# Attention by halves of a batch, woven into the chunks, and the token mix from chunk 7 on

## The chip, the cores and the metric

The kernel runs on one core of a Trainium2 chip. The metric is the device time of one execution in microseconds (us), the median of several runs; lower is better. TensorE (PE) does the matrix products, VectorE (DVE) and ScalarE (ACT) work on what it leaves in PSUM, GpSimd (POOL) has no PSUM work here, and SyncE (SP) issues every DMA.

## The reference, cut to what matters

Four batches of 576 tokens; 8 heads of 64 columns.

```python
scores = q @ k.T / sqrt(64)                      # per batch and head, 576 x 576
rel = pos[:, None] - pos[None, :]
plain   = (rel >= 0) & (rel < 32)                # heads 0 to 3
dilated = (rel >= 0) & (rel < 128) & (rel % 4 == 0)   # heads 4 to 7
attn = softmax(where(mask, scores, -1e9)); x = attn @ v          # B, S, 512

xk = mu_k * x + (1 - mu_k) * x_prev; xr = mu_r * x + (1 - mu_r) * x_prev   # first block
x2 = sigmoid(xr @ w_r) * (relu(xk @ w_k) ** 2 @ w_v)             # 512 -> 1024 -> 512

u = x2 + (x2.T @ U @ V).T                        # second block: token mix, rank 32
out = u + relu(u @ w_ch1) @ w_ch2                # 512 -> 2048 -> 512
```

Only 32 keys count for a query. A dilated head is a plain one once the tokens are sorted by their residue mod 4 (144 tokens each).

## The kernel before, in words

**Precision.** Every large product is done as three passes: each operand is split into a high part (a copy to fp32r) and a low part (value minus high part), and `three` (L1083 to L1087) issues high*high, low*high and high*low. The weights arrive by DMA in pieces of 512 KB in staging buffers; ACT makes the high part (`split_high`, L690) and POOL the low part (`split_low`, L544). The ten pieces of the first block are needed from chunk 0 on. `x` is kept with the 512 features on partitions, 4 groups of 128, 2304 tokens along.

**Attention.** A pair of heads of one batch goes through four stages. A: transposes of q and k to features on partitions (L1108); ACT drains q into `q_t`, where both heads' queries lie interleaved and zeros stand at the other head's rows, DVE drains k. B: scores, 9 units of 64 queries by 96 keys (L1115); one matmul has 128 stationary columns, 64 queries of both heads. DVE adds the mask and takes the maximum (L889, L893), ACT takes the exponentials one unit at a time (L676), DVE normalises (`normalise`, L913). C: transposes of the probabilities (L1121), drained by ACT (L667). D: products with v, one matmul per head with 64 stationary columns (L1129), drained by DVE into `x`. ORDER (L56) lists the 16 steps of one batch. Four PSUM banks are used in turn.

**First block.** Nine chunks of 256 tokens. A chunk has ten units (L83): eight of kind k (12 matmuls of 256 columns) and two of kind r (12 matmuls of 512 columns), and eight groups v (6 matmuls of 512 columns), placed by V_AFTER. Between its units stand the slots for other work. During chunk c the inputs of chunk c+1 are made: `shift` on ACT, `mix` on DVE for k, `make_xr` on POOL for r; `high_x` on ACT makes the high parts, `low_xk` on DVE and `low_xr` on POOL the low ones. At the end of a chunk DVE multiplies the result with the sigmoid (L1018).

**Order of work.** All of it is written out by hand, and every engine runs its list in order. First the whole attention of batch 0, with ACT and POOL splitting the ten pieces. Then three turns of a loop: chunks 2i and 2i+1, with the 16 steps of batch i+1 in 16 of their 20 slots. Chunks 6, 7 and 8 have the token mix in their slots (X_SLOT, G_SLOT, H_SLOT, L120): U and V are split on POOL (L576 to L593) after its work for chunk 6, and the first two pieces of the second block are split by ACT between chunks 6 and 7 (L820), by POOL after its work for chunk 7.

**Second block.** Six chunks of 384 tokens, 16 units each; nothing in it is touched.

**DMA.** SP issues in one list: q and k of a pair with 6 DMAs, v of a plain pair with 4 and of a dilated one with 13 (L428 to L432, one for each run of keys of one residue), and a piece when its staging buffer, one of three, is free.

Of the kernel before, what the change touches and what calls it, by code (L numbers as in the profile page):

```python
# [45 lines left out]
NU = S // UQ  # L46
# [6 lines left out]
FULL = S_FULL * P  # L53
# [4 lines left out]
PARTS = {"A": 3, "B": 2, "C": 3, "D": 3}  # L58
B_UNITS = [range(0, 5), range(5, NU)]
CD_UNITS = [range(0, 3), range(3, 6), range(6, 9)]  # L60
SPLIT_SLOT = [1, 2, 4, 5, 6, 8, 9, 11, 12, 13]
NORM_SLOT = {4: 0, 6: 1, 9: 2, 12: 3}
GROUPS = [(st, p, j) for st, p in ORDER for j in range(PARTS[st])]
GROUP = {key: n for n, key in enumerate(GROUPS)}
NG = len(GROUPS)
# [3 lines left out]
def drained_by_scalar(key):  # L69
    return key[0] == "C" or (key[0] == "A" and key[2] < 2)  # L70


SCALAR_N = [sum(drained_by_scalar(k) for k in GROUPS[:n + 1]) for n in range(NG)]
VECTOR_N = [n + 1 - SCALAR_N[n] for n in range(NG)]
SCALAR_ALL, VECTOR_ALL = SCALAR_N[-1], VECTOR_N[-1]
# [10 lines left out]
NUNIT = len(UNITS)  # L86

SIGMOID_SLOT = {"early": [(4, 0, 0), (5, 0, 1), (5, 0, 2), (5, 0, 3), (7, 1, 0), (7, 1, 1), (NUNIT, 1, 2), (NUNIT, 1, 3)],
                "late": [(4, 0, 0), (4, 0, 1), (4, 0, 2), (4, 0, 3), (7, 1, 0), (8, 1, 1), (NUNIT, 1, 2), (NUNIT, 1, 3)],
# [3 lines left out]
SHIFT_SLOT = {"early": [1, 1, 3, 3], "late": [3, 3, 4, 6]}  # L93
MIX_SLOT = {"early": [2, 2, 5, 5], "late": [4, 4, 6, 7]}
# [24 lines left out]
LATE = 3 * NUNIT  # L119
# [30 lines left out]
def dilated_runs():  # L150

    runs = []
    for i in range(NU):
        a, end = max(UQ * i - WINDOW, 0), UQ * i + UQ
        while a < end:
            r, j = divmod(a, SUB)
            n = min(end - a, SUB - j)
            runs.append((i, a - (UQ * i - WINDOW), n, r, j))
            a += n
    return runs  # L160


DIL_RUNS = dilated_runs()
V_PLAIN, V_DIL = 4 * 16, len(DIL_RUNS) * 16
V_BATCH = V_PLAIN + V_DIL
QK_LOADS = 6 * 16


def build(nc, q, k, v, mu_k, mu_r, w_k, w_v, w_r, u_in, v_in, w_ch1, w_ch2, out):
    ctx = ExitStack()  # L170
    with ctx:
# [18 lines left out]
        q_raw = [sb(f"q_raw{n}", [P, S_TILES, P], c=first) for n in range(2)]  # L190
        k_raw = [sb(f"k_raw{n}", [P, S_TILES, P], c=first) for n in range(2)]
        v_raw = [sb(f"v_raw{n}", [UK, NU, P], c=first) for n in range(2)]
        q_t = sb("q_t", [P, S, 2], c=first)
        k_t = sb("k_t", [P, WINDOW + S], c=first)
        probs = [sb(f"probs{n}", [P, NU, UK], c=first) for n in range(2)]
        probs_t = sb("probs_t", [UK, NU, P], c=first)
        masks = sb("masks", [P, 2, NU, UK], BF16, c=first)
        neg_max = sb("neg_max", [P, 2, NU], c=first)
        sums = sb("sums", [P, 2, NU], c=first)
        inv = sb("inv", [P, 2, NU], c=first)  # L200
# [30 lines left out]
        x2_h = sb("x2_h", [P, 2, D], F32R, c=third)  # L231
# [6 lines left out]
        sb("rest_of_token_mix", [P, 4 * D + B * D + 2 * (DH + S + DH) - 4 * WPIECE], c=second)  # L238
# [18 lines left out]
        qk_in = [sem(f"qk_in{n}") for n in range(2)]  # L257
        values_in = [sem(f"values_in{n}") for n in range(2)]
        mu_in = sem("mu_in")
        stage_in = [sem(f"stage_in{n}") for n in range(3)]  # L260
        u_zero = sem("u_zero")
        consts = sem("consts")
        pool_own = sem("pool_own")
# [52 lines left out]
        def shifted_ready(eng, kind, c, t, start, zeroed_here):  # L316

            wait(eng, (shift_k, shift_r)[kind], KT * c + t + 1)  # L320
            if start is not None:
                eng.tensor_copy(shifted[:, kind, HEAD_PAIR[t], bass.ds((S - 2 * C1) * (start + 1), 1)], zeros[:, :])\
                    .then_inc(zeroed_here, 1)
                wait(eng, zeroed_here, KT * start + t + 1)


        CREDIT = {id(unit_out): 2, id(sqh_done): 2, id(sql_done): 2, id(v_mm): 4, id(x2_done): 2,
                  id(hl_done): 2, id(o_mm): 4, id(fin): 1, id(out_done): 16}
# [986 lines left out]
```

## Time and profile before

| | us |
|---|---|
| median of three runs (lowest, highest) | 828.92 (828.72, 829.6) |
| the profiled execution | 828.38 |
| its span, first to last instruction | 826.6 |
| PE busy | 790.1 (96%) |
| ACT, DVE, POOL busy | 337.3, 370.5, 138.3 |

The times in the rows of the next sections count from the start of the span. "Idle before" is the time for which the engine stood still just before an instruction, with what released it. The profiled execution lies 1.8 us above its span and 0.5 us under the median.

### The profile page before, as it was taken

What the parts mean: (1) busy time and instruction counts of PE and PEld (TensorE: products, weight loads), DVE (VectorE), ACT (ScalarE), POOL (GpSimd) and SP (SyncE); (2) the same over time, 40 slices, a digit from 0 to 9 for tenths busy, and PEclk for the clock granted to TensorE, in tenths of its full rate; (3) what the DMA queues carried; (4) which work ended last, traced back from release to release, by engine and by line L of the source; (5) the groups of instructions that cost most, each with busy time, mean ns of one, the idle gap of its engine ahead of it and who ended that gap; (6) DMA issues with size and microseconds to landing.
All of it is one profiled execution on the core that took longest, in us unless ns stands there. A gap on an engine that the chain in (4) does not pass through costs nothing.

```text
span 826.6 us, 13887 instructions
## 1 busy us (share of the span) xinstructions
PE 790.1 (96%) x4848; PEld 703.5 (85%) x4848; DVE 370.5 (45%) x675; ACT 337.3 (41%) x879; POOL 138.3 (17%) x121
## 2 busy tenths in 40 slices
PE   6569999999999999799999999999999999999998
PEld 5458888888889888588889999999989999989997
DVE  3564968596768688877731131131112113113111
ACT  4888865886587755543333211111111101111110
POOL 4462012102211141311066400000000000000000
PEclk9859999999999999899999999999999999999999
DMA  6763121303030100100033110010000000001001
GB/s 156 198 162 79 38 63 38 78 21 82 20 74 21 42 27 26 51 1 2 1 128 128 52 39 1 0 39 0 0 0 38 0 0 38 0 0 38 1 1 39
DMA packets 82435, 35.53 MB, mean 43 GB/s; under 512 B 70240, under 2 KB 76384, under 8 KB 82400
## 3 DMA queue, kind: packets, MB, share of 16 engines
q1 hardware_dynamic: 82400, 35.07, 15.4%
q8 instruction: 21, 0.34, 0.2%
q14 instruction: 14, 0.11, 0.0%
HBM read 30.33 MB, written 4.72 MB: 42 GB/s over the span
## 4 chain that ended last, share of the span: by engine, by line
PE 90%; ACT 3%; DVE 3%; SPq 1%; issue 1%; DMA 1%; POOL 0%; ACTq 0%; DVEq 0%
PE bank L1085 26%; PE bank L1087 26%; PE bank L1086 26%; PE bank L1115 4%; PE bank L1129 2%; PE bank L1108 2%; PE bank L1121 2%; ACT probs L676 1%; PE bank L1161 1%; SPq L431 1%; PE bank L1219 1%; PE bank L1233 1%; PE bank L1220 1%; ACT probs_t L667 1%; PE bank L1234 0%
## 5 line engine op out<-in xcount | busy, mean ns | idle before, releaser
L1054 DVE SCALAR_TENSOR_TENSOR h_l<-bank,h_h 128x384 fp32r<-128x384 f32 x96 | 53.5, 558 | 308.9 <-ACT h_h L837 308.9
L837 ACT ACTIVATE h_h<-bank 128x384 fp32r<-128x384 f32 x96 | 47.3, 492 | 333.0 <-PE bank L1087 333.0
L1085 PE MATMUL bank<-ut_h,w_h 128*128 128x384 f32 x384 | 130.4, 340 | 0.0
L1087 PE MATMUL bank<-ut_h,w_l 128*128 128x384 f32 x384 | 129.2, 337 | 0.0
L1086 PE MATMUL bank<-ut_l,w_h 128*128 128x384 f32 x384 | 128.8, 335 | 0.0
L1087 PE MATMUL bank<-w_h,h_l 128*128 128x512 f32 x288 | 113.7, 395 | 0.0
L1086 PE MATMUL bank<-w_l,h_h 128*128 128x512 f32 x288 | 113.5, 394 | 0.0
L1085 PE MATMUL bank<-w_h,h_h 128*128 128x512 f32 x288 | 111.9, 389 | 0.0
L1085 PE MATMUL bank<-xs_h,wk_h 128*128 128x256 f32 x288 | 84.4, 293 | 3.3 <-DVE xs_l L1040 2.8
L1086 PE MATMUL bank<-xs_l,wk_h 128*128 128x256 f32 x288 | 81.1, 282 | 0.0
L1087 PE MATMUL bank<-xs_h,wk_l 128*128 128x256 f32 x288 | 81.0, 281 | 0.0
L1085 PEld LDWEIGHTS bank<-ut_h,w_h 128*128 128x128 f32 x384 | 72.2, 188 | 3.1
L1086 PEld LDWEIGHTS bank<-ut_l,w_h 128*128 128x128 f32 x384 | 72.2, 188 | 3.1
L1087 PEld LDWEIGHTS bank<-ut_h,w_l 128*128 128x128 f32 x384 | 72.0, 188 | 0.0
L770 ACT ACTIVATE relu_k<-bank 128x256 f32<-128x256 f32 x72 | 27.9, 387 | 101.1 <-PE bank L1087 100.8
L1087 PEld LDWEIGHTS bank<-w_h,h_l 128*128 128x128 f32 x288 | 54.0, 187 | 11.5
L961 DVE RECIPROCAL sig<-sig 128x128 f32<-128x128 f32 x72 | 63.4, 922 | 0.6
L1085 PE MATMUL bank<-wv_h,sq_h 128*128 128x512 f32 x144 | 57.8, 402 | 4.8 <-DVE sq_l L951 4.8
L1086 PEld LDWEIGHTS bank<-w_l,h_h 128*128 128x128 f32 x288 | 54.0, 188 | 9.4
L1085 PEld LDWEIGHTS bank<-w_h,h_h 128*128 128x128 f32 x288 | 54.1, 188 | 9.0
L1085 PEld LDWEIGHTS bank<-xs_h,wk_h 128*128 128x128 f32 x288 | 54.9, 190 | 6.2 <-DVE xs_l L1040 3.0
L1086 PE MATMUL bank<-wv_l,sq_h 128*128 128x512 f32 x144 | 57.4, 398 | 0.0
(121 smaller groups left out, 1376.9 us busy)
## 6 DMA issues: line engine op xcount, KB each, us to landing
stage<-in_moe_w_ch_dram SPq DMA_DIRECT2D x16, 512.0 KB, 3.2
out_dram<-result SPq DMA_DIRECT2D x18, 256.0 KB, 2.1
q_raw<-in_q_dram SPq DMA_DIRECT2D x32, 128.0 KB, 2.4
k_raw<-in_k_dram SPq DMA_DIRECT2D x32, 128.0 KB, 2.4
v_raw<-in_v_dram SPq DMA_DIRECT2D x16, 144.0 KB, 2.6
stage<-in_moe_w_k_dram SPq DMA_DIRECT2D x3, 512.0 KB, 3.9
v_raw<-in_v_dram SPq DMA_DIRECT2D x32, 48.0 KB, 1.8
stage<-in_moe_w_r_dram SPq DMA_DIRECT2D x2, 512.0 KB, 5.2
```

Source lines behind the costliest of these rows:

```text
L431: sp.dma_start(dst[row:row + n, i, :].rearrange("p (h d) -> p h d", h=2), rows[r, j:j + n]).then_inc(landed, 16)
L770: act.activation(relu_k[:, m % 2, :], unit_bank[n % 2][:, 0:C1], ACT.Relu).then_inc(unit_out, 1)
L837: act.activation(h_h[:, m % KRING, :], h_bank[m % 2][:, 0:C2], ACT.Relu).then_inc(hh_done, 1)
L961: dve.reciprocal(sig[:, t, cols], sig[:, t, cols]).then_inc(sig_done, 1)
L1054: dve.scalar_tensor_tensor(h_l[:, m % KRING, :], h_bank[m % 2][:, 0:C2], 0.0, h_h[:, m % KRING, :].bitcast(F32), op0=ALU.max, op1=ALU.subt ...
L1085: pe.matmul(dst, lhs[0], rhs[0], start=start, stop=False)
L1086: pe.matmul(dst, lhs[0], rhs[1], start=False, stop=False)
L1087: return pe.matmul(dst, lhs[1], rhs[0], start=False, stop=stop)
L1108: ins = pe.transpose(dst[:, t * P:t * P + P], (qr if j == 0 else kr)[:, t, :], ident[:, :])
L1115: ins = pe.matmul(dst[:, n * UK:n * UK + UK], q_t[:, i * UQ:i * UQ + UQ, :].rearrange("p a b -> p (a b)"), k_t[:, i * UQ:i * UQ + UK], sta ...
L1121: ins = pe.transpose(dst[0:UK, n * P:n * P + P], probs[p % 2][:, i, :], ident[:, :])
L1129: ins = pe.matmul(dst[rows, n * UQ:n * UQ + UQ], v_raw[p % 2][:, i, rows], probs_t[:, i, UQ * h:UQ * h + UQ], start=True, stop=True)
```

## The change

- A batch is cut at token 256: part 2b has 256 tokens, part 2b+1 has 320. Attention goes part by part (8 parts, 4 pairs each). Only part 0 and three steps of part 1 (A and B of pair 0, A of pair 1) come before chunk 0; parts 1 to 7 are woven into chunks 0 to 6 (`steps_in`), the steps of part c+1 in chunk c. The loop over batches is gone: every chunk is written out.
- Dilated pairs: within a part the four residues are four units (64 keys in an even part, 96 in an odd one), and the last 64 queries of the odd part are one unit against 192 keys.
- `q_t` holds the heads apart; a score unit is two matmuls with 64 stationary columns each, that write partitions 0 to 63 and 64 to 127.
- v of a dilated pair takes 2 or 6 DMAs. Three buffers each for q, k and v. Two staging buffers for pieces in place of three.
- POOL makes both parts of the ten pieces (`split_both`), six of them, then a third mask, then `make_xr(0)`, then the other four. Low parts in two halves.
- The slots of `shift` and `mix` are the same in each chunk (2, 4, 6, 8 and 3, 5, 7, 9). Normalising stands in the slot of stage C.
- The token mix takes the slots of chunks 7 and 8. On POOL the splits of U and V come after `make_xr(7)`.

```diff
-ORDER = [("A", 0), ("B", 0), ("A", 1), ("B", 1), ("A", 2), ("C", 0), ("B", 2), ("D", 0), ("A", 3), ("C", 1),
-         ("B", 3), ("D", 1), ("C", 2), ("D", 2), ("C", 3), ("D", 3)]
-NORM_SLOT = {4: 0, 6: 1, 9: 2, 12: 3}
+BEFORE = [("A", 0, 0), ("A", 0, 1), ("B", 0, 0), ("A", 0, 2), ("B", 0, 1), ("C", 0, 0), ("D", 0, 0), ("A", 0, 3), ("B", 0, 2),
+          ("C", 0, 1), ("D", 0, 1), ("B", 0, 3), ("C", 0, 2), ("D", 0, 2), ("A", 1, 0), ("C", 0, 3), ("D", 0, 3),
+          ("B", 1, 0), ("A", 1, 1)]
+def steps_in(slot):
+    out = []
+    for k in range(1, NPART):
+        for p in range(PAIRS):
+            start = NUNIT * (k - 1) - 3 + 2 * p
+            out += [(st, k, p) for st, after in (("D", 4), ("A", 0), ("C", 3), ("B", 1)) if start + after == slot]
+    return sorted(out, key=lambda step: "DACB".index(step[0]))
-SHIFT_SLOT = {"early": [1, 1, 3, 3], "late": [3, 3, 4, 6]}
-MIX_SLOT = {"early": [2, 2, 5, 5], "late": [4, 4, 6, 7]}
+SHIFT_SLOT = [2, 4, 6, 8]
+MIX_SLOT = [3, 5, 7, 9]
-X_SLOT = [*range(1, 13), 13, 14, 21, 22, LATE, LATE]
+X_SLOT = [1, 1, 2, 3, 4, 4, 5, 6, 7, 7, 8, 9, 10, 10, 11, 12, LATE, LATE]
-H_SLOT = [*range(8, 21), *[LATE + 3] * (NTILE - 13)]
+H_SLOT = [7, 8, 9, 9, 10, 11, 12, 13, 13, 14, 15, 16, 17] + [LATE + 3] * (NTILE - 13)
...
             def load_piece(n):
-                if 3 <= n < NB_PIECES:
-                    sp.wait_ge(w_split, n - 2)
-                elif n >= NB_PIECES:
+                if n >= 2:
                     sp.wait_ge(w_split, n - 1)
...
             load_qk(0, 0)
-            load_qk(1, 0)
+            load_qk(0, 1)
+            load_v(0, 0)
+            load_qk(0, 2)
             load_piece(0)
-            load_qk(2, 0)
+            load_v(0, 1)
             load_piece(1)
...
+            load_qk(0, 3)
+            load_v(0, 2)
+            load_qk(1, 0)
+            load_piece(2)
+            load_v(0, 3)
+            load_qk(1, 1)
             load_piece(3)
+            load_v(1, 0)
             load_piece(4)
+            load_qk(1, 2)
             load_piece(5)
...
+            def split_both(n):
+                raw, hi, lo = piece(n)
+                pool.wait_ge(stage_in[slot_of(n)], STAGE_COUNT[n])
+                half = raw.shape[1] // 2
+                for a in (slice(0, half), slice(half, 2 * half)):
+                    step(pool.tensor_copy(hi[:, a], raw[:, a]))
+                    ins = pool.tensor_tensor(lo[:, a], raw[:, a], hi[:, a].bitcast(F32), ALU.subtract)
+                ins.then_inc(w_split, 1)
+            EARLY1 = 6
+            for n in range(EARLY1):
+                split_both(n)
+            step(pool.memset(mask_ends[:, :, :], 0.0))
+            for h in range(2):
+                part, runs = mask_ends[UQ * h:UQ * h + UQ, :, :], UQ // DILATION
+                keep(part, 0, [[-runs, DILATION], [0, UK // 2]], 1)
+                keep(part, runs - 1, [[runs, DILATION], [0, UK // 2]], -1)
+                keep(part, -1, [[runs, DILATION], [1, UK // 2]], -1)
+                keep(part, WINDOW, [[-runs, DILATION], [-1, UK // 2]], 1)
+            pool.sem_inc(masks_done, 1)
...
             make_xr(0)
-            with pool.Fori(0, B - 1) as i:
-                make_xr(2 * i + 1)
-                make_xr(2 * i + 2, start=i)
+            for n in range(EARLY1, NB_PIECES):
+                split_both(n)
+            pool.wait_ge(w_split, NB_PIECES)
+            pool.memset(stage[PIECE_U % 2][:, 0:2 * S_TILES * RANK], 0.0).then_inc(u_zero, 1)
+            for c in range(1, NC1 - 1):
+                make_xr(c)
...
-            make_xr(NC1 - 2)
             split_low(FIRST2)
             split_low(FIRST2 + 1)
             make_xr(NC1 - 1)
...
+            for c in range(NC1):                      # ScalarE
+                if c == NC1 - 2:
+                    split_high(FIRST2)
+                    split_high(FIRST2 + 1)
+                chunk(c)
...
                 elif stage_ == "B":                   # VectorE
+                    if n >= 2:
+                        wait_mm(dve, last_bank("C", *divmod(n - 2, PAIRS)))
+                    wait(dve, masks_done, 3 if dil and half else 1 if dil else 2)
...
+                    if c < MIX_CHUNK:                 # VectorE, chunk(c), before the sigmoids
+                        slot = c * NUNIT + n
+                        for k, p in [(k, p) for st, k, p in steps_in(slot) if st == "C"]:
+                            normalise(k, p)
...
-                        for n, i in enumerate(B_UNITS[j]):        # TensorE, stage B
-                            ins = pe.matmul(dst[:, n * UK:n * UK + UK], q_t[:, i * UQ:i * UQ + UQ, :].rearrange("p a b -> p (a b)"),
-                                            k_t[:, i * UQ:i * UQ + UK], start=True, stop=True)
+                            for h in range(2):
+                                out_ = dst[DH * h:DH * h + DH, col:col + keys]
+                                if keys == 2 * UK:
+                                    out_ = out_.rearrange("p (r j) -> p r j", r=DILATION)
+                                ins = pe.matmul(out_, q_t[n % 2][:, h, query:query + UQ], rhs, start=True, stop=True)
```

ACT's order inside a chunk is: drain of unit n, square, then `exps` part 0 of the pair whose B was in the slot before, the drains of this slot's steps, `exps` part 1, then `shift`. ACT no longer splits the first ten pieces.

## Rows read from the trace of the kernel before

**Rows 1.** The page: the span in 40 slices, busy tenths of PE.
```profile
PE   6569999999999999799999999999999999999998
```

**Rows 2.** Stretches: length, busy us of each engine (instructions), clock, DMA share, GB/s.
```profile
0.00:63.20 63.20, 36.52 (x292) 31.20 (x292) 31.57 (x61) 45.98 (x132) 33.71 (x29) 0.78 0.65 170
143.50:222.80 79.30, 79.02 (x630) 70.07 (x629) 58.67 (x118) 56.94 (x170) 12.07 (x15) 1.00 0.23 51
302.10:333.80 31.70, 31.70 (x185) 27.55 (x183) 25.33 (x41) 19.77 (x44) 11.38 (x14) 1.00 0.10 34
333.80:345.00 11.20, 5.92 (x22) 4.56 (x22) 11.06 (x8) 2.04 (x4) 7.16 (x3) 0.70 0.27 94
```

**Rows 3.** Timelines of SP's queue and of ACT, start-up: start, us, engine line.
```profile
8.09 0.60 SPq L451 DMA_DIRECT2D stage<-in_moe_w_k_dram  x1
10.48 1.15 SPq L402 DMA_DIRECT2D k_raw<-in_k_dram  x2
28.57 6.88 SPq L431 DMA_DIRECT2D v_raw<-in_v_dram  x13
...
12.00 1.06 ACT L694 ACTIVATE wk_h<-stage 128x1024 fp32r<-128x1024 f32 x1 [2.59 <-DMA stage<-in_moe_w_k_dram]
```

**Rows 4.** POOL: two groups by form (busy us, mean ns), and one timeline row.
```profile
L548 POOL TENSOR_TENSOR w_l<-stage,w_h 128x1024 fp32r<-128x1024 f32 x16 | 38.6, 2413 | 53.1 <-ACT w_h L694 53.1
L603 POOL COPY u_tile<-x 128x512 f32 x12 | 7.3, 617 | 200.6 <-PE bank L1161 200.6
...
6.91 1.01 POOL L536 TENSOR_SCALAR_AFFINE_SELECT masks<-masks 128x48 bf16<-128x48 bf16 x3
```

**Rows 5.** Timeline of PE in chunk 0: scores and v products, and what follows each.
```profile
91.90 2.14 PE L1115 MATMUL bank<-k_t,q_t 128*128 128x96 f32 x18
93.82 0.36 PE L1085 MATMUL bank<-xs_h,wk_h 128*128 128x256 f32 x1
...
95.40 1.27 PE L1129 MATMUL bank<-probs_t,v_raw 96*64 96x64 f32 x36
96.60 0.39 PE L1085 MATMUL bank<-xs_h,wk_h 128*128 128x256 f32 x1
```

**Rows 6.** Timeline of PE and DVE where chunk 3 ends and chunk 4 begins.
```profile
222.62 0.40 PE L1087 MATMUL bank<-wv_h,sq_l 128*128 128x512 f32 x1
222.85 0.28 PE L1085 MATMUL bank<-xs_h,wk_h 128*128 128x256 f32 x1
222.97 0.28 PE L1086 MATMUL bank<-xs_l,wk_h 128*128 128x256 f32 x1
...
223.68 1.29 DVE L1018 TENSOR_TENSOR x<-bank,sig 128x512 f32 x2
```

**Rows 7.** Timelines around 335: DVE, POOL, PE (in brackets: idle before, releaser).
```profile
333.95 2.31 DVE L947 TENSOR_TENSOR sq<-relu_k 128x256 f32<-128x256 f32 x1
336.29 2.44 DVE L951 TENSOR_TENSOR sq_l<-sq,sq_h 128x256 fp32r<-128x256 f32 x1
...
335.93 5.04 POOL L548 TENSOR_TENSOR w_l<-stage,w_h 128x1024 fp32r<-128x1024 f32 x2
...
338.79 0.79 PE L1085 MATMUL bank<-wv_h,sq_h 128*128 128x512 f32 x1 [4.80 <-DVE sq_l L951]
```

**Rows 8.** ACT and DVE groups by form, and exponentials in the chain of waits.
```profile
L647 ACT ACTIVATE q_t<-bank 64x512 f32<-64x512 f32 x32 | 20.0, 624 | 6.7 <-PE bank L1108 6.5
L921 DVE TENSOR_TENSOR probs<-probs,inv 128x864 f32<-128x864 f32 x16 | 16.9, 1058 | 0.5
...
16.73 1.78 ACT probs L676 x10
```

**Rows 9.** Timeline of POOL where chunk 6 begins: first and last of its splits.
```profile
301.02 2.51 POOL L559 TENSOR_TENSOR xs_l<-xf,xs_h 128x1024 fp32r<-128x1024 f32 x1 [6.71 <-ACT xs_h L727]
303.47 0.46 POOL L579 CAST u_split<-stage 128x320 fp32r<-128x320 f32 x1
308.66 1.49 POOL L592 TENSOR_TENSOR vp_l<-stage,vp_h 128x576 fp32r<-128x576 f32 x1
```

More of the change, by code:

```diff
@@ new lines, with banks_of @@
+NUNIT = 10
+def steps_in(slot):
[5 more added lines that the diff above has]
+    return sorted(out, key=lambda step: "DACB".index(step[0]))
+LAST_SLOT = NUNIT * (NPART - 2) - 3 + 2 * (PAIRS - 1) + 4
+PE_STEPS = BEFORE + [step for slot in range(LAST_SLOT + 1) for step in steps_in(slot)]
+def banks_of(step):
+    st, k, p = step
+    if st == "A":
+        return 2
+    if st == "B":
+        return 2 if DILATED[p] and k % 2 else 1
+    if st == "C":
+        return 1 + k % 2
+    return 1
@@ L64, with last_bank @@
+GROUPS = [(st, k, p, j) for st, k, p in PE_STEPS for j in range(banks_of((st, k, p)))]
 GROUP = {key: n for n, key in enumerate(GROUPS)}
-NG = len(GROUPS)
-ABANKS = 4
+def last_bank(st, k, p):
+    return (st, k, p, banks_of((st, k, p)) - 1)
 def drained_by_scalar(key):
[L70 to L75, printed above, removed]
+    return key[0] == "C" or (key[0] == "A" and key[3] == 0)
@@ L78, with part_for @@
+SCALAR_N = [sum(drained_by_scalar(k) for k in GROUPS[:n + 1]) for n in range(len(GROUPS))]
+VECTOR_N = [n + 1 - SCALAR_N[n] for n in range(len(GROUPS))]
+LAST_D = ("D", NPART - 1, PAIRS - 1, 0)
+def part_for(c):
+    return min(c, NPART - 1)
 C1 = 256
@@ L147, in mix_steps, with build @@
     return steps
[L150 to L169, printed above, removed]
+def build(nc, q, k_in, v, mu_k, mu_r, w_k, w_v, w_r, u_in, v_in, w_ch1, w_ch2, out):
     ctx = ExitStack()
@@ new lines, in exps @@
+            def exps(k, p, part):
+                n = nth(k, p)
+                b = n % 2
+                wait(act, maxed, n + 1)
+                every = list(enumerate(units(k, p)))
+                for i, (_, col, keys) in (every[:2], every[2:])[part]:
+                    ins = act.activation(probs[b][:, col:col + keys], probs[b][:, col:col + keys], ACT.Exp,
+                                         bias=neg_max[:, b, i:i + 1], accum_out=sums[:, b, i:i + 1])
+                if part:
+                    ins.then_inc(exped, 1)
@@ L690, in split_high, with attention_slot @@
+            def attention_slot(slot):
+                behind = [(k, p) for st, k, p in steps_in(slot - 1) if st == "B"] if slot else []
+                for k, p in behind:
+                    exps(k, p, 0)
+                for step in steps_in(slot):
+                    attention(*step)
+                for k, p in behind:
+                    exps(k, p, 1)
             def split_high(n):
@@ new lines, in attention @@
+                        for i, (col, keys) in enumerate(cols[4 * j:4 * j + 4]):
+                            ins = pe.transpose(dst[0:keys, i * P:i * P + P], probs[n % 2][:, col:col + keys], ident[:, :])
+                    else:
+                        pe.wait_ge(values_in[n % VALUES], V_COUNT[n])
+                        wait_drained(pe, last_bank("C", k, p))
+                        for i, (query, _, keys) in enumerate(units(k, p)):
+                            blocks = max(1, keys // UK)
+                            for a in range(blocks):
+                                for h in range(2):
+                                    rows, kk = slice(DH * h, DH * h + DH), min(keys, UK)
+                                    ins = pe.matmul(dst[rows, query:query + UQ], v_raw[n % VALUES][0:kk, i + a, rows],
+                                                    probs_t[n % 2][0:kk, i + a, rows], start=a == 0, stop=a == blocks - 1)
@@ L1163, in turn, with chunk @@
                 ins.then_inc(t_mm, 1)
[L1165 removed]
+            def chunk(c):
+                last = c == NC1 - 1
                 for n, (kind, m) in enumerate(UNITS):
```

716 lines of the change are left out of this document (350 added, 366 removed).

## The prediction, made before the changed kernel was timed

> **What bounds the kernel now.** I read the page first: PE is busy in nine tenths or more of nearly every slice except the first three and one near 340 [rows 1]. Then the stretches, for what the start costs: until 63.2 us PE works 36.5 us at a mean clock of 0.78, and the pair of chunks from 143.5 to 222.8 has it busy 79.0 of 79.3 us at full clock [rows 2]. So TensorE bounds everything behind 63.2, and 826.6 - 63.2 = 763.4 us come after it. There are two places to win. The start: its chain of waits runs through SP's queue, the exponentials and the splits; SP needs 0.58 us for each DMA of q or k and 6.88 us for the 13 of one dilated v [rows 3]. And the stretch 333.8 to 345.0: 22 matmuls that at full speed, 0.12 us for 256 columns and 0.23 for 512 [rows 6], take about 3.5 us last 11.2 us at a clock of 0.70 [rows 2]. That costs 7.7 us. Its first part is an idle time of 4.80 us behind DVE's `sq_l` [rows 7].
>
> **The start.** The first dense matmul comes at T, now 63.2. Part 0 is 256 of 576 tokens, ACT is rid of ten casts, and the dilated v of half a batch takes 2 DMAs. I estimate from the stage times that the attention of part 0 would be done near 42. But DVE's work for B of part 1, pair 0 waits for the third mask, which POOL makes after six pieces, and `mix` of the last feature group, the last exponentials and the last high and low part come behind it in the engines' order. So POOL and SP set T.
>
> SP in its new order: 14 DMAs, piece 0, 2, piece 1, 14 + 2 for mu, piece 2, 10, piece 3, 6, piece 4, 6, piece 5. At 0.58 to 0.6 us each they are issued at about 9, 11, 21, 28, 32 and 36 us. A piece issued at 8.09 was used at 12.00 [rows 3], so they land 3.9 us later. POOL per piece: two copies of 128x512 at 0.62 [rows 4]; two subtractions of half of 128x1024, 2.41 for the whole, so 1.2 to 1.3 each [rows 4]; two gaps of 0.1. That is 4.0 us. Pieces done at 17, 21, 29, 35.5, 39.5, 44. The third mask is nine steps; three selects take 1.01 us [rows 4], with 192 columns a little more, so 4 us: 48 (45 if SP takes 0.5 us for the 64 KB loads). Behind it: DVE's two adds and two maxima of 576 columns in all, 1.9 (864 columns take 1.06 once [rows 8]); five exponentials 1.9 (five take 1.78 [rows 8]); ACT's drain of A 1.2; `shift` 0.4, `mix` 0.5, high and low 0.9. That is 7.0 us. T = 52 to 55; I take 54.
>
> **Work that moves behind T.** One batch of attention costs PE 79.3 - 2 x 28.0 = 23.2 us (28.0: 96 matmuls x 0.117 + 72 x 0.233 [rows 6]). Part 1 is 320/576 of it, 12.9; three of its steps, 2.5, stay in front. +10.4. So at T = 54 the start has gained 9.2 and paid 10.4.
>
> **Scores.** A unit takes 1.92/9 = 0.21 us, start to start; the 18 products of D with 64 stationary columns take 1.20, 0.033 for each of 36 instructions [rows 5]. The new unit has four instructions with 96 columns moving. Below: 0.033 each, 0.13 a unit. Above: 0.08 each if two halves never overlap, 0.32. I take 0.17, near D's row scaled by 96/64, since D has the same shape of output: 126 units woven x -0.04 = -5 us (range -10 to +13). Dilated pairs have ten blocks for nine in C and D: 14 x 0.13 = +1.9. Twice as many steps, half as long: each visit costs PE about 0.1 (after B the next matmul starts 0.2 later for 0.12 [rows 5, 6]), and 56 more steps +5.
> The Trainium skill (TensorEngine Tiling (Array Packing), Key Properties) says that changing the tiling mode drains TensorE; here D's neighbours show no more than 0.1 to 0.2 us, and by that the new B adds only what stands above. The same section says that different tiles can load and multiply in parallel, and D's row agrees.
>
> **Waits in the woven chunks.** In each chunk two places have a chain longer than PE's cover. PE is in order, so they are paid each time.
> (a) Slot 4. PE does A of pair 3 in slot 3, then one k unit of 1.4 us, then C of pair 2. ACT's list between is: drain q of A (2 x 0.40, between half of 0.62 and the whole [rows 8]), then the second part of pair 2's exponentials, 2 or 3 x 0.36 [rows 8], then DVE's `normalise`, 0.2 + 0.25 + 0.5 or 0.6 (1.06 for 864 columns [rows 8]). That is 2.65 to 3.25 with the hops against 1.75: 0.9 or 1.4 in each of seven chunks, 8.6 us.
> (b) Slot 0. `normalise` of the next pair 0 stands on DVE behind the two products at L1018, which wait for PE's last v: from there 1.29 [rows 6] + 0.9 to 1.3, against one k unit of 1.4: 1.1 or 1.5 at six boundaries, 7.5 us; in the row DVE starts them only 0.8 us after the chunk's end [rows 6], and the wait would be larger by that. Together 16; I take 15.
>
> **The stall at 334** arose where POOL worked 128x1024 subtractions back to back: DVE's 256-column products took 2.31 and 2.44 us for 0.42 otherwise [rows 7]. In the new order POOL's two follow its U and V work, not the end of a chunk. -7.7.
> The Trainium skill (SBUF, Who interferes with whom) says that a VectorE instruction with two SBUF inputs and a GpSimd one that reads SBUF lock each other out for a whole instruction. The rows agree. It speaks against this change.
>
> **A new wait before chunk 7.** ACT splits the second block's first two pieces there, as before. Their DMAs wait for the splits of U and V, which now come after `make_xr(7)`, at the end of chunk 6, where they came a chunk earlier. From the chunk's start S (302.13, [rows 9] around it): POOL's low part until S + 1.3, U and V from 303.47 to 310.15, thus V at S + 8.0 [rows 9]; SP and landing 3.9; cast 1.0: ACT is back at S + 12.9. PE has two banks, so it does k0 and k1 until S + 2.8 and then stands until S + 13.2. 10.4, and some 2 more at half clock, as behind the idle time at 338.8. +12.5.
>
> **Chunk 0.** POOL splits four pieces from T + 7 to T + 24, while DVE has its squares and `normalise` there. Some 17 two-input operations each wait 0.6 on average: 10 us on an engine with 6 us of slack. Between 0 and 8; +2. The r unit's inputs come at T + 7, when PE gets there at T + 8: nothing. Chunks 7 and 8 hold the token mix of three: DVE about 31 of PE's 36 us, nothing.
>
> **The sum.** 54 + 763.4 + 10.4 + 1.9 + 5 - 5 - 7.7 + 12.5 + 2 + 15 = 851.5 us of span; the profiled execution was 1.8 over its span, and the median 0.5 over that: 853.8.
>
> **Rivals.**
> 1. *The weave hides all, and the start is bound by the attention.* No wait in (a), (b) or chunk 0, and T = 42: 853.8 - 17 - 12 = 825, faster. For it: the loop before has PE at 99.6% with 58.7 and 56.9 of 79.3 us on DVE and ACT [rows 2]. Against: before, `normalise` had slots of its own ahead of C, and the mask's place is in the code. It decides from T below 46.
> 2. *T as computed, no waits in the woven chunks*: 838.8. For it: the same row; a longer slot elsewhere than I read.
> 3. *POOL's splits lock DVE out.* If each contended operation of DVE in the start and in chunk 0 costs 1.2 us, as the hold of a half subtraction, T rises by 4 and chunk 0 by 8: 866.
> 4. *The two halves of a score unit don't overlap* (0.32 a unit): 872.
>
> **Chances.** The forecast's case 0.62 (its own range 840 to 867), rival 1 0.12, rival 2 0.14, rival 3 0.08, rival 4 0.04. A measurement of this kernel can tell about 0.2% from none. Faster: rival 1 with a mixture of it and 2, 0.14; within 0.2%, 0.03; slower 0.83. The range 832 to 868 leaves rival 1, rival 4 and the ends.
>
> **What would show it.** First `wk_h` matmul at 52 to 56, with DVE's B of part 1 released by POOL's mask. In each of chunks 0 to 6 a wait of PE at a transpose of stage C behind `normalise`, 0.9 to 1.5 us, one in slot 4, one in slot 0. In chunk 7 an idle time of PE near 10 us behind ACT's `relu_k` or exponential, ACT waiting for the DMA of a `stage`. Score instructions near 0.042 us each. No idle time behind `sq_l` at the end of chunk 6. It is wrong if T lies near 42, if PE's share in the woven chunks stays at 99%, or if ACT doesn't wait for the piece.

## The result, and the profile after

The changed kernel takes 893.42 us (median of 4 runs, 888.86 to 897.48) against 829.26 for the kernel before on the same chip: a ratio of 1.0772, 95% interval [1.0717, 1.0828]. I had forecast 853.8 and a range that ended at 868. The sign was right and the size was not.

The profiled execution is the fastest of the four (888.86 us, span 887.1), 4.6 us under the median. So all the accounts from traces below explain the 60.5 us between the two profiled spans, and not the 64.2 between the medians. Its page: busy tenths of PE in 40 slices of 22 us, and the clock granted to it.

```profile
PE   4558998999989898959799999999999999999998
...
PEclk9969999999999999979999999999999999999999
```

Against [rows 1], eights now stand between the nines up to the sixteenth slice, then a five where chunk 7 begins and a seven where it ends. The last 416.3 us, from the second block's start at 470.77, are as long as before (from 410.28); so all of the +60.5 us lies ahead of that point. The stretches from one chunk's start to the next, chunks 0 to 8 (length, busy us of each engine with instructions, clock, DMA share, GB/s):

```profile
55.25:102.86 47.61, 44.30 (x374) 36.89 (x375) 34.61 (x65) 31.02 (x95) 24.14 (x26) 0.96 0.29 71
102.86:148.37 45.51, 42.12 (x337) 34.83 (x336) 31.58 (x68) 26.03 (x84) 6.17 (x9) 0.96 0.23 52
148.37:195.13 46.76, 42.39 (x375) 35.21 (x374) 33.28 (x68) 28.36 (x89) 5.11 (x5) 1.00 0.17 39
...
332.90:377.96 45.06, 40.70 (x352) 33.88 (x350) 31.67 (x64) 25.98 (x76) 6.29 (x6) 1.00 0.08 17
377.96:430.86 52.90, 39.47 (x202) 32.95 (x200) 33.31 (x50) 23.77 (x49) 17.63 (x16) 0.87 0.12 41
430.86:470.77 39.91, 37.00 (x213) 32.01 (x212) 27.08 (x47) 11.67 (x26) 0.00 (x0) 1.00 0.00 1
```

A pair of woven chunks, 1 and 2, takes 92.27 us; its counterpart took 79.3 with PE busy for 79.0 [rows 2]. In each of these woven chunks PE now stands still for some 3.4 or 4.4 us. What it waited for, from the first dense matmul on (us in total, times, longest):

```profile
PE bank L1198 <- DVE probs L984: 16.1, 10, 2.1
PE bank L1153 <- DVE xs_l L1095: 12.1, 1, 12.1
PE bank L1198 <- DVE probs L987: 10.5, 4, 3.1
PE bank L1153 <- ACT relu_k L814: 9.1, 1, 9.1
PE bank L1309 <- DVE x L1031: 6.9, 2, 4.0
```

The first and third are the waits of stage C in the woven chunks, 26.6 us in fourteen waits, where I had 15 and 2. The second is the start's own: it ends at T. The fourth is the wait before chunk 7. The fifth is in the token mix (4.0 in chunk 7, 2.9 in chunk 8), and I had forecast nothing there.

Where one chunk becomes the next, DVE and POOL (start, length, instruction):

```profile
148.57 1.29 DVE L1086 TENSOR_TENSOR x<-bank,sig 128x512 f32<-128x512 f32 x2 [0.15 <-PE bank L1155]
149.78 2.01 DVE L979 TENSOR_SCALAR sums<-sums 128x5 f32<-128x5 f32 x1
151.82 0.19 DVE L981 RECIPROCAL inv<-sums 128x5 f32<-128x5 f32 x1
152.05 0.56 DVE L984 TENSOR_TENSOR probs<-probs,inv 128x384 f32<-128x384 f32 x1
152.53 0.35 DVE L987 TENSOR_TENSOR probs<-probs,inv 128x192 f32<-128x192 f32 x1
```

```profile
149.41 2.36 POOL L620 TENSOR_TENSOR xs_l<-xf,xs_h 128x1024 fp32r<-128x1024 f32 x1 [7.36 <-ACT xs_h L771]
```

An addition to five columns lasts 2.01 us, for 0.17 elsewhere, and ends when POOL's subtraction of 128x1024 ends (151.77). PE waits behind it and then answers with C, B and dense work:

```profile
153.02 0.83 PE L1198 MATMUL bank<-ident,probs 128*96 128x128 f32 x6 [3.08 <-DVE probs L987]
153.78 1.21 PE L1192 MATMUL bank<-k_t,q_t 128*64 128x96 f32 x20
```

Before chunk 7, ACT waits for a stage that POOL's splits of U and V have freed late, and PE waits for ACT and then runs at the lower level of its clock (512 columns start 0.43 apart, for 0.23):

```profile
385.18 1.06 ACT L738 ACTIVATE w_h<-stage 128x1024 fp32r<-128x1024 f32 x1 [8.49 <-DMA stage<-in_moe_w_ch_dram]
388.67 1.06 ACT L738 ACTIVATE w_h<-stage 128x1024 fp32r<-128x1024 f32 x1 [2.43 <-DMA stage<-in_moe_w_ch_dram]
389.63 0.37 ACT L814 ACTIVATE relu_k<-bank 128x256 f32<-128x256 f32 x1
```

```profile
390.05 0.79 PE L1153 MATMUL bank<-wr_h,xs_h 128*128 128x512 f32 x1 [9.13 <-ACT relu_k L814]
390.64 0.63 PE L1154 MATMUL bank<-wr_l,xs_h 128*128 128x512 f32 x1
```

### The profile page after: what moved, and what is told of

Its sections match the earlier page's. It is cut to its first block, busy times and chain, and to the rows that moved or that the text cites. A ratio compares the mean times of both kernels' runs of the same rounds, so it can differ in the third digit from the quotient of the medians.

```text
span 887.1 us, 13661 instructions
## 1 busy us (share of the span) xinstructions
PE 808.1 (91%) x5176; PEld 699.0 (79%) x5176; DVE 390.9 (44%) x750; ACT 317.3 (36%) x869; POOL 150.7 (17%) x168
## 4 chain that ended last, share of the span: by engine, by line
PE 83%; DVE 8%; ACT 3%; issue 2%; POOL 2%; SPq 1%; DMA 1%; DVEq 0%; POOLq 0%; ACTq 0%
PE bank L1153 24%; PE bank L1154 23%; PE bank L1155 23%; PE bank L1192 3%; PE bank L1207 3%; PE bank L1198 2%; PE bank L1169 2%; DVE sums L979 1%; DVE probs L984 1%; DVE x L1086 1%; PE bank L1236 1%; ACT probs L720 1%; SPq L446 1%; DVE sig L1021 1%; ACT xs_h L771 1%
## 5 line engine op out<-in xcount | busy, mean ns | idle before, releaser
L1153 PE MATMUL bank<-xs_h,wk_h 128*128 128x256 f32 x288 | 87.6, 304 | 12.1 <-DVE xs_l L1095 12.1
L1153 PEld LDWEIGHTS bank<-xs_h,wk_h 128*128 128x128 f32 x288 | 56.0, 194 | 17.6 <-DVE xs_l L1095 12.3
L720 ACT ACTIVATE probs<-probs,neg_max 128x96 f32<-128x96 f32 (+1 forms) x144 | 52.0, 363 | 20.9 <-DVE neg_max L957 11.1
```

What stands on the lines that cost most here:

```text
L720: ins = act.activation(probs[b][:, col:col + keys], probs[b][:, col:col + keys], ACT.Exp, bias=neg_max[:, b, i:i + 1], accum_out=sums[:, b ...
L1153: pe.matmul(dst, lhs[0], rhs[0], start=start, stop=False)
```

## The experiments

All but experiment 8 are edits to the changed kernel. Times are medians of four runs (five in experiment 8), ratios are to the kernel before on the same chip, and "less" is against the 893.42 of the change. The chips are not all the same one: the kernel before took 828.77 to 830.11 on them. The median of the change lies 4.6 us above its profiled execution, so "less" by medians can be more than the traces show; where it matters, the difference between the profiled spans (887.1 for the change) stands beside it.

**1. The wait before chunk 7.** ACT casts the second block's first two pieces after units 4 and 5 of chunk 7, no longer ahead of it.

```diff
-                if c == NC1 - 2:
-                    split_high(FIRST2)
-                    split_high(FIRST2 + 1)
                 chunk(c)
...
+                        if c == MIX_CHUNK and n in (4, 5):
+                            split_high(FIRST2 + n - 4)
```

> ScalarE casts the second block's first two pieces after units 4 and 5 of chunk 7 and not ahead of chunk 7; the rest is as in the changed kernel. Theory (ScalarE stands for the two DMAs, 8.49 and 2.43 us, and PE with it): PE's wait of 9.13 us behind relu_k goes, and 1.8 us of half clock behind it: chunks 7 and 8 together 92.8 us before, 82 now, the run 11 us shorter, 877 us of span. The waits at the token mix (4.02 and 2.91 us) stay, as they hang on the order of the lists at the end of chunk 7. Rival (the cast is only one of several late things, GpSimd's list is the real one): PE's wait turns up again within chunk 7 behind GpSimd's late inputs of chunk 8, and less than 5 us are won.

Measured: 880.77, ratio 1.0632 [1.0608, 1.0657]; 12.7 less, or 9.8 from one profiled span to the other. Chunk 7 went from 52.90 to 42.53 us and the wait behind `relu_k` is gone from the list. The cause is shown, at nearly the price forecast for it (12.5 in the prediction, 11 in the expectation, 10.4 in the chunk here).

**2. Normalise before the chunk's last product.** DVE normalises the next pair 0 before it waits for the last v.

```diff
+                if c + 1 < MIX_CHUNK:
+                    normalise(c + 2, 0)
                 wait(dve, v_mm, (c + 1) * M1)
```

> VectorE normalises pair 0 of the next part before the two products at a chunk's end that wait for PE's last v, not behind them; the rest is as in the changed kernel. Theory (order of VectorE's list plus GpSimd's lock on the shared port): the wait of PE at stage C in slot 0, 2.14 us for even and 3.08 us for odd parts at six boundaries, 15.7 us, goes to under 0.3 us each, and the small addition of 4 or 5 columns, 1.3 to 2.0 us now, takes 0.2 us again, as it runs ahead of GpSimd's low part. The run is 15 us shorter or some more, as the wait for probs_t in slot 1 (0.8 us, four times) goes too. Rival (VectorE and ScalarE are simply overloaded in the woven chunks): the wait moves to the next stage of the chain, and less than 5 us are won.

Measured: 875.49, ratio 1.0547 [1.0529, 1.0564]; 17.9 less by medians, 10.0 between the profiled spans, of which this one is the slowest of its four (15 expected). The waits at slot 0 of odd parts, 3.08 each, are gone altogether; those of even parts fell from 2.14 only to 1.71. The DVE rows say why: the multiplication itself is now the one that is held, beside POOL's subtraction (192.47 to 194.84).

```profile
192.17 0.10 DVE L979 TENSOR_SCALAR sums<-sums 128x4 f32<-128x4 f32 x1
...
192.53 2.59 DVE L984 TENSOR_TENSOR probs<-probs,inv 128x256 f32<-128x256 f32 x1
```

**3. POOL out of DVE's way.** POOL's `low_xr` waits until that normalisation is done; DVE's list stays as it is.

```diff
                 wait(pool, xh_done, 2 * c + 2)
+                if 1 <= c < MIX_CHUNK:
+                    wait(pool, normed, nth(c + 1, 0) + 1)
```

> GpSimd's 128x1024 subtraction of chunks 1 to 6 waits until pair 0 is normalised; VectorE's order is that of the changed kernel. Theory (the addition of 4 or 5 columns stands 1.1 to 1.8 us for GpSimd's instruction): it takes 0.2 us again, and the wait of PE in slot 0 falls from 2.14 and 3.08 us to about 1.1 and 1.4 us, which is what the working without the lock gave; 8 us shorter over six boundaries. Rival (the time of the small addition has another cause, as the wait for the exponentials): it stays at 1.3 to 2.0 us, and nothing is won; or the r unit now waits for GpSimd and gives it back.

Measured: 875.84, ratio 1.0556 [1.0538, 1.0574]; 17.6 less where I expected 8. The waits at slot 0 are 0.99 and 1.23, for 2.14 and 3.08 (I had forecast 1.1 and 1.5). The same place in its trace:

```profile
146.62 1.29 DVE L1088 TENSOR_TENSOR x<-bank,sig 128x512 f32<-128x512 f32 x2
147.83 0.16 DVE L981 TENSOR_SCALAR sums<-sums 128x5 f32<-128x5 f32 x1
...
148.25 0.56 DVE L986 TENSOR_TENSOR probs<-probs,inv 128x384 f32<-128x384 f32 x1
```

The addition takes 0.16 us when POOL stands still. The six waits are shorter by 3 x 1.15 and 3 x 1.85, 9.0 us, and the clock has 4.4 more. T came 0.7 later in this run. That makes the 12.8 between the profiled spans; the other 4.8 of the 17.6 lie between medians and profiled executions. Chunks 2 and 3 of this kernel as one stretch:

```profile
146.43:234.21 87.78, 83.03 (x711) 68.66 (x710) 61.91 (x135) 54.27 (x171) 11.26 (x14) 1.00 0.21 48
```

Chunks 1, 3 and 5 of the change had a mean clock of 0.96; here none of the six has. In chunk 1 of the change PE waited until 106.56 and was then granted 0.57 of its clock for 3 us:

```profile
102.86:106.56 3.70, 1.57 (x13) 1.38 (x12) 3.39 (x6) 1.22 (x3) 2.37 (x1) 1.00 0.04 10
106.56:109.50 2.94, 2.94 (x26) 2.58 (x27) 1.06 (x3) 0.59 (x1) 0.00 (x0) 0.57 0.03 6
109.50:112.00 2.50, 2.50 (x29) 2.30 (x29) 1.03 (x3) 1.08 (x5) 0.00 (x0) 0.82 0.00 0
```

Such a fall costs about 1.5 us, in three chunks 4.4: chunk 1 with the same waits took 44.04 us at clock 1.00 in experiment 1 and 45.51 at 0.96 in the change. It is not bound to one wait: in the change it follows the 2.14 of odd chunks and not the 3.08 of even ones, and in experiment 4 it follows the 3.08 of chunk 2 (48.28 us for 46.76). When it comes is open.

**4. The masks earlier.** POOL makes `mask_ends` before its small pieces.

```diff
+            step(pool.memset(mask_ends[:, :, :], 0.0))
+            for h in range(2):
+                part, runs = mask_ends[UQ * h:UQ * h + UQ, :, :], UQ // DILATION
...
+            pool.sem_inc(masks_done, 1)
+
             def split_low(n):
```

> GpSimd makes the third mask with the other two, ahead of the six pieces; the rest is as in the changed kernel. Theory (the first dense matmul, now at 55.25 us, hangs on that mask, which is done at 48.6): the attention of part 0 is through at 42, and the first dense matmul comes at 49 to 50. The run is 5 to 6 us shorter. Pieces 0 to 5 come up to 4 us later on GpSimd where they don't wait for DMA; the sixth by less than 2 us. Rival (the attention chain or the pieces would hold chunk 0 anyway): the first dense matmul stays above 53, or PE waits for the r piece in unit 2 and gives the gain back.

Measured: 886.7, ratio 1.0696 [1.0675, 1.0718]; 6.7 less by medians, 3.6 between the profiled spans: four woven chunks of this trace (2, 4, 5 and 6) have a mean clock of 0.96, for three in the change. The first dense matmul came at 49.36 (the wait ahead of it 5.4 for 12.1). The mask is what held the start from 49.4 to 55.25.

**5. Exponentials before A.** ACT does all exponentials of a pair before it drains the next A.

```diff
                 for k, p in behind:
                     exps(k, p, 0)
+                    exps(k, p, 1)
                 for step in steps_in(slot):
                     attention(*step)
```

> ScalarE takes all exponentials of a pair before it drains the slot's steps; the rest is as in the changed kernel. Theory (the wait of PE in slot 4 is the chain A of pair 3, drain, second part of the exponentials, normalise, C of pair 2): with the exponentials ahead, the wait of 1.25 to 1.28 us at six of the seven places goes to under 0.3 us, and the 2.08 us of chunk 0 to about 1. 8 us shorter. The slot 0 wait stays or falls by at most 0.4. Rival (VectorE's own work bounds the chain there): the slot 4 wait stays above 1 us.

Measured: 892.89, ratio 1.0767 [1.0751, 1.0784]: nothing gained. The wait of slot 4 fell only from 1.25 to 0.95 (1.28 to 0.87). In its trace ACT's last exponential ends at 123.90, but DVE, now later with `k_t`, still has the square and its low part ahead of the normalisation:

```profile
124.30 0.42 DVE L929 COPY k_t<-bank 128x256 f32<-128x256 f32 x1
124.64 0.41 DVE L1006 TENSOR_TENSOR sq<-relu_k 128x256 f32<-128x256 f32 x1
125.09 0.42 DVE L1010 TENSOR_TENSOR sq_l<-sq,sq_h 128x256 fp32r<-128x256 f32 x1
125.44 0.16 DVE L978 TENSOR_SCALAR sums<-sums 128x4 f32<-128x4 f32 x1
```

I had named ACT's list as the cause in (a). It was one of two lists of nearly the same length, and taking one away uncovered the other. The theory fell as a cause; its price of 0.9 and 1.4 had come out near. The 0.3 and 0.4 that were won in each chunk don't show in the time: in this trace the clock fell in chunks 1, 2, 5 and 6 (0.96, 0.93, 0.96, 0.93).

**6. Scores as 128-column tiles again**, two heads side by side in one stationary tile, half as many instructions.

```diff
-                            for h in range(2):
-                                out_ = dst[DH * h:DH * h + DH, col:col + keys]
+                            out_ = dst[:, col:col + keys]
...
-                                ins = pe.matmul(out_, q_t[n % 2][:, h, query:query + UQ], rhs, start=True, stop=True)
+                            ins = pe.matmul(out_, q_t[n % 2][:, query // UQ, :, :].rearrange("p h c -> p (h c)"), rhs,
+                                            start=True, stop=True)
```

> A score unit is one matmul with 128 stationary columns, both heads, as before the change; q_t keeps the two heads of a unit side by side. The rest is as in the changed kernel. Theory (the scores as 64-column tiles save almost nothing, 1.88 us a pair and part-pair against 1.95, and each entry into and out of a 64-column layout costs PE 0.1 to 0.2 us): the stages B take 0.07 us more for each pair of a batch, but C followed by B falls by 0.18 us, 28 times; the run is between 2 and 5 us shorter. Rival (my forecast: 64-column tiles save 0.04 us a unit): the run is 5 us longer.

Measured: 890.88, ratio 1.0751 [1.0735, 1.0768]; 2.5 less, about what such runs differ by. A stage B of this kernel and the same of the change (both in chunk 2, both at full clock):

```profile
162.98 1.25 PE L1195 MATMUL bank<-k_t,q_t 128*128 128x96 f32 x10
164.01 0.36 PE L1157 MATMUL bank<-xs_h,wk_h 128*128 128x256 f32 x1
```

```profile
163.58 1.05 PE L1192 MATMUL bank<-k_t,q_t 128*64 128x96 f32 x20
164.56 0.38 PE L1153 MATMUL bank<-xs_h,wk_h 128*128 128x256 f32 x1
```

Start to start it is 1.03 us for ten wide tiles and 0.98 for twenty narrow ones; the even halves take 0.81 either way. Two 64-column tiles do overlap, so rival 4 is out, and together they cost what one of 128 columns costs. The -5 us of my sum has nothing behind it; if anything the wide form is the cheaper one, by less than this run can tell.

**7. The tails of A side by side.** The transposes of the 64-row tails follow each other, where whole and tail tiles alternated.

```diff
-                        for t in range(2):
-                            ins = pe.transpose(dst[:, t * P:t * P + P], raw[:, t, :], ident[:, :])
-                        if half:
-                            ins = pe.transpose(dst[:, WHOLE:WHOLE + TAIL], raw[0:TAIL, 2, :], ident[0:TAIL, 0:TAIL])
+                        for t in ((0, 1, 2) if j == 0 else (2, 0, 1))[j and not half:2 + (half or j)]:
+                            if t == 2:
+                                ins = pe.transpose(dst[:, WHOLE:WHOLE + TAIL], raw[0:TAIL, 2, :], ident[0:TAIL, 0:TAIL])
+                            else:
+                                ins = pe.transpose(dst[:, t * P:t * P + P], raw[:, t, :], ident[:, :])
```

> In stage A of the odd parts the two 64-row transposes of the tails stand next to each other (q 0, q 1, q tail, k tail, k 0, k 1); the rest is as in the changed kernel. Theory (a change of the array's layout costs PE 0.1 us or so): stage A of an odd part, 1.14 us now, falls to about 0.95 us, 16 times; 2 to 4 us shorter. Rival (the tail itself costs 0.3 us, wherever it stands): 1.14 us as now.

Measured: 893.72, ratio 1.0782 [1.0765, 1.0798]: no gain. Stage A of an odd part did fall, from 1.14 us to 0.83, and a chunk at full clock from 44.04 (experiment 1) to 43.35. But the waits of the even chunks grew by 0.33 each, since PE came earlier to a DVE that did not, and the falls of the clock that came here (0.93 in chunks 2 and 4) took the rest. PE time ahead of a wait is not worth its length.

**8. The kernel before without its stall at 334.** POOL's `low_xr` of that chunk waits until DVE's `low_xk` is done.

```diff
                 wait(pool, xh_done, 2 * c + 2)
+                if isinstance(c, int) and c == NC1 - 2:
+                    wait(pool, xkl_done, c + 1)
```

> The kernel before the change, with one wait more: GpSimd's low part of xr for chunk 7, and with it its two subtractions for the second block's pieces, waits until VectorE's low part of xk for chunk 7 is done. Theory (the stall at 333.8 to 345.0 is GpSimd's three 128x1024 subtractions holding VectorE's sq, sq_l and xs_l): sq and sq_l take 0.42 us there, PE's wait of 4.80 us goes, and chunk 6 ends near 335.3 instead of 342.2; the run is 6 to 7.7 us shorter, 821 to 823 us. Rival (VectorE is late there for its own load): the wait stays. Or GpSimd's later work meets the first squares of chunk 7 and PE waits there: 2 to 4 us won.

Measured: 823.96 (823.2 to 826.2) against 828.77, ratio 0.9941 [0.9927, 0.9954]: 4.8 less, where I expected 6 to 7.7. Chunk 6 takes 34.2 us for 40.1; POOL's subtractions now lie behind DVE's squares:

```profile
337.03 0.41 DVE L949 TENSOR_TENSOR sq<-relu_k 128x256 f32<-128x256 f32 x1
337.48 0.42 DVE L953 TENSOR_TENSOR sq_l<-sq,sq_h 128x256 fp32r<-128x256 f32 x1
...
342.45 2.04 DVE L986 TENSOR_TENSOR x_l<-x,x_h 128x512 fp32r<-128x512 f32 x1 [0.34 <-ACT x_h L750]
```

```profile
344.54 0.50 PE L1221 MATMUL bank<-x_h,u_split 128*128 128x512 f32 x1 [1.18 <-DVE x_l L986]
```

The two products that took 2.31 and 2.44 us [rows 7] take 0.41 and 0.42. PE still waits 0.90 us behind the second, at 337.96, and another operation of DVE takes the hold at 342.45: it lasts 2.04 us for 0.69, and PE waits 1.18 us behind it. So part of the stall moved into chunk 7, which takes 38.0 us for 37.4, as the expectation's last rival had it. (The profiled spans differ by only 2.2 us, since the first dense matmul of this run, the slowest of its five, came at 65.98 for 63.24.) This one line is a version that beats both kernels, by little but clear of the noise, and most of what the change gains at 334 is had without the change.

**9. Edits 1 to 4, 6 and 7 together.**

> All six edits at once: the two weight pieces cast by ACT behind units 4 and 5 of chunk 7, probabilities normalised ahead of chunk end's multiply, POOL's low_xr behind that normalisation, masks built before the small pieces, scores as 128-column tiles, the tails transposed side by side. Theory (the loss is waits in the woven chunks, the clock that falls with them, the wait before chunk 7, and 3.8 us of PE per batch more than before): first dense matmul at 49.4; a pair of woven chunks 83.0 - 1.3 (tails) + 3.1 (waits left: slot 0 of even parts 0.6, slot 4 1.25 and 1.28) = 84.8 instead of 92.3; chunk 7 42.5 instead of 52.9; second block after 49.4 + 46 + 3 x 84.8 - 1.7 + 42.5 + 39.9 = 431; time 431 + 416.3 + 1.8 = 849, 846 to 852, still slower than before (829), since what PE itself does more (part 1's share moved 10.4, 3.5 x 2.5 of switching and of small steps) stays. Rival (the clock falls by itself in about every second woven chunk, whatever the waits): each such chunk 1.5 us longer, 855 to 860. Rival (the gains overlap: they are one wait seen three times): 865 to 870.

Measured: 852.35 (850.9 to 852.97), ratio 1.0271 [1.0254, 1.0288]. The first dense matmul comes at 49.55. Chunks 1 and 2 as one stretch, and what PE still waits for:

```profile
99.34:183.64 84.30, 81.05 (x639) 70.68 (x638) 61.41 (x135) 54.17 (x171) 11.37 (x14) 1.00 0.22 49
```

```profile
PE bank L1207 <- DVE probs L989: 10.2, 7, 1.6
PE bank L1318 <- DVE x L1036: 6.6, 2, 3.6
...
PE bank L1207 <- DVE probs L992: 3.3, 4, 2.2
```

84.3 for the pair (84.8 expected), and the clock stands at 1.00 in all six woven chunks: it doesn't fall by itself in each second chunk, and rival one is out. Edits 2 and 3 shorten the same wait (17.9 and 17.6 alone) and count once; with that the gains add, 12.7 + 17.9 + 6.7 + 2.5 - 0.3 = 39.5 by medians against 41.1 here, so rival two is out as well. The time is 0.35 over my range's end; the miss is in chunk 0, 49.8 us for the 46 I had put down, with waits of 2.20 and 1.62. The rest of it is PE's speed: it is busy for 45.97 us there and for 41.51 in chunk 2, which also weaves an odd part. Products of 256 columns start 0.21 us apart at the chunk's beginning, for 0.12 elsewhere:

```profile
50.14 0.41 PE L1163 MATMUL bank<-xs_h,wk_l 128*128 128x256 f32 x1
50.35 0.41 PE L1161 MATMUL bank<-xs_h,wk_h 128*128 128x256 f32 x1
```

That is the spacing of the clock's lower level, and it ends near 55.5, though the column of the granted clock reads 1.00 for this stretch. Behind the wait of 2.20 the column reads 0.50 for 2 us (66 to 68).

**10. Together, and the token mix ahead of the next chunk's cast.** ACT takes `x_h` of chunk 7's last unit before `high_x`.

```diff
-                        if n == NUNIT - 1 and not last:
+                        if n == NUNIT - 1 and not last and c < MIX_CHUNK:
                             high_x(0, c + 1)
...
                             mix_step(*step)
+                        if n == NUNIT - 1 and not last:
+                            high_x(0, c + 1)
```

> As together, and ACT takes the token mix's x_h of the last unit of chunk 7 before high_x of the next chunk's xk instead of behind it. Theory (the wait of 4.0 us before L1309 at the end of chunk 7 is x_h queued behind a 1.06 us cast that waits for DVE's last xf): that wait falls by 1.1 to 1.3 us, the time by 1 to 2 us against together; the wait of 2.9 us at the start of chunk 8 stays. Rival (the wait is DVE's own list, x_l, g_split, x one behind the other): no change within 0.3 us.

Measured: 852.67 (848.92 to 855.82), ratio 1.0269 [1.0230, 1.0308]: by time no difference that can be told. By the trace, the wait fell from 3.65 to 2.69 and chunk 7 from 42.38 to 41.61, a little less than I expected, so the order on ACT is a quarter of that wait. Of the other 2.7, 2.1 are DVE's own list, x_l, g_split and x one behind the other (383.59 to 385.73), and the rest lies ahead of it, with ACT's `x_h`. In the change that stands so:

```profile
422.44 0.69 DVE L1046 TENSOR_TENSOR x_l<-x,x_h 128x512 fp32r<-128x512 f32 x1 [1.64 <-ACT x_h L792]
423.16 0.69 DVE L1040 TENSOR_TENSOR g_split<-bank,g_split 64x512 fp32r<-64x512 f32 x1
423.89 0.69 DVE L1031 TENSOR_TENSOR x<-bank,x 128x512 f32<-128x512 f32 x1
```

```profile
424.63 0.80 PE L1309 MATMUL bank<-g_split,vp_h 128*128 128x512 f32 x1 [4.02 <-DVE x L1031]
```

## Why the prediction was wrong, by its own steps

Up to the second block I had forecast 851.5 - 826.6 = +24.9 us, and +60.5 were measured. Step by step, forecast and measured:

| Step | forecast | measured | from |
|---|---|---|---|
| The start (T) | -9.2 | -8.0 | T 55.25, forecast 54 |
| Part 1's share moved behind T | +10.4 | taken as it was | not measured apart |
| Waits of stage C, chunks 0 to 6 | +17 | +26.6 | list of waits |
| Clock in chunks 1, 3, 5 | 0 | +4.4 | 3 x 1.47 |
| PE's own work for attention, each batch more | +1.9 | +13 to +14 | 3.5 x (83.0 - 79.3, or 79.0) |
| Wait before chunk 7 | +12.5 | +10.9 | 9.13, and 1.75 of slow clock |
| Stall at 334 | -7.7 | -7.7 | no wait behind `sq_l` |
| Token mix | 0 | +9 | 6.9 of waits, 1.6 to 2 of slow clock |

The measured column sums to 58.6 to 59.6 of 60.5; the remainder is not assigned, and I put nothing on it. Against the forecast the largest misses are PE's own work (11 to 12), the waits of stage C (9.6), the token mix (9) and the clock (4.4).

**What held.** T, and what sets it: DVE's B of part 1 began at 48.67, released by POOL, whose last mask select ended at 48.5, and experiment 4 moved T by moving the mask. The wait of ACT for a stage, its place and its size (experiment 1). The stall that goes. Waits at both places of each woven chunk, (a) at 1.25 and 1.28 for 0.9 and 1.4.

**Step (b) failed in its size.** I had 1.1 and 1.5 at slot 0; it was 2.14 and 3.08. I had listed DVE's chain from the chunk's end as multiplications and small operations at their undisturbed lengths, and had not asked what POOL does at that moment. POOL's `low_xr` stands just there in each chunk. Experiment 3 takes POOL away and finds 0.99 and 1.23, my own numbers; so the chain was right and the missing term is the hold, 1.2 to 1.9 us each time. I had written the hold down as rival 3, but only for the start and chunk 0, where POOL has the splits. The row to look at was there: POOL's 2.51 us at 301.02, just before the start of chunk 6 at 302.13 [rows 9]; there it costs nothing, since nothing that it holds lies beside it. DVE's two reciprocals and the products at L1018 keep their lengths through it, as the kernel before shows:

```profile
301.17 1.76 DVE L961 RECIPROCAL sig<-sig 128x128 f32<-128x128 f32 x2
302.96 1.29 DVE L1018 TENSOR_TENSOR x<-bank,sig 128x512 f32 x2
```

The change put the small addition there, which is held.

**The steps for PE's own work failed.** "-5" for the scores, "+5" for the visits and "+1.9" for the tenth block made +1.9; the measured +3.7 to +4.0 a batch make +13 to +14. Experiment 3's stretch and [rows 2] show it at the same clock with no wait counted: PE busy 83.0 against 79.0. The scores gain nothing (experiment 6); the 20 instructions in 0.98 us are 0.049 each, for the 0.042 I had put down. 1.2 us a pair of chunks is the alternation of whole and tail tiles in A (four stages of odd parts at 0.31, experiment 7). With that and the wide scores 81.05 are left (experiment 9), 2.0 over before, 2.0 x 3.5 = 7 for all. I put it down to the shorter steps and the more visits, for which I had +5 and +1.9, and that is near; no run takes it apart. What failed is the -5, and the alternation in A, 1.2 x 3.5 = 4, which had no term.

**Two things weren't in the sum.** The token mix: I had checked that DVE's busy time fits into PE's, 31 of 36 us, which says nothing of the order in which three engines hand a tile on. And the clock: I counted it behind the long wait before chunk 7, and not behind short ones.

**Of the rivals**, 1 and 2 are out by the waits, and 4 by the length of stage B (0.98 us for five units, where it asked for 1.6). Rival 3 had the right mechanism in the wrong place: it wanted 4 us more at the start and 8 in chunk 0, where T came 1.25 later than forecast and the waits were 3.3 us; the price was paid at each chunk's border.

**Where the weave stands.** With the six edits of experiment 9 it takes 852, still 23 us more than before: T is 13.7 us earlier (49.55 for 63.24) and 7.7 are gained at 334, but 10.4 of attention moved behind T, 13.5 us of waits at stage C are left, PE does 7 us more of its own, and 7.6 go in the token mix. That makes 17 of the 22.5 us between the two spans. Most of the rest lies in chunk 0, where PE is busy 4.5 us longer than in chunk 2, with its instructions spaced as at the lower clock (experiment 9); the kernel before takes only 1 us more for its chunk 0 than for its chunk 2 (44.2 and 43.1). These are chains of three engines, B, maximum, exponential, normalise, C, that got half as much dense work to hide behind. That a cut by halves can't be made to win isn't shown; no variant run here did.

## What to carry to other kernels

When a loop runs with its bounding engine at 99.6% and a step is cut in half, list for each place where the engine waits the whole chain in the other engines' order, and beside it what every engine that shares memory access with them does in the same microseconds; a small instruction in a chain can cost what its neighbour's large one lasts. A sum of busy times that fits proves no handover. And before moving work to win back a stall, try the one-line edit that removes the stall: here the kernel before won 0.6% by letting one subtraction, and what stands behind it on POOL, wait.

## What the runs showed of the hardware

A VectorE addition of a scalar to 128x5 values, one input, took up to 2.01 us beside a GpSimd subtraction of 128x1024, and 0.16 without it. I had expected this only of instructions with two inputs. Not every VectorE instruction is held: two reciprocals of 128x128 took their usual 1.76 us beside the subtraction at 301.02 in the kernel before. The Trainium skill (SBUF, Who interferes with whom) counts `tensor_scalar` among the operations that can enter modes that use the shared ports; the run agrees that it can be held, and the operation at hand is too small to show in which mode it was.

Two scores tiles of 64 columns, 20 instructions in 0.98 us, cost as much as ten of 128 columns in 1.03. Whole and 64-row transposes in turn took 1.14 us for six, and 0.83 with equal ones side by side.

A wait of 2.14 us of TensorE was followed by 3 us at 0.57 of its clock in one chunk, and a wait of 3.08 in the next by none; runs of one and the same kernel differ by up to 8.6 us (888.86 to 897.48), while the kernel whose waits are shorter, experiment 3, keeps within 0.9. That the clock is what makes them differ fits with the mean clocks of those four runs, 0.979, 0.983, 0.970 and 0.981 for 888.86, 891.99, 897.48 and 894.85, but only roughly.
